# Attention by head pairs in a three-stage fp32 program: probabilities leave PSUM once, the product with V runs as plain fp32 on two column strips, and three stages share one block

## The reference, cut to what matters

```python
# q, k, v: [4 batches, 8 heads, 576, 64]
x = (log1p(|i - j|) / log1p(max(i, 1)))[..., None]
bias = maximum(x @ w1 + b1, 0) @ w2            # [576, 576, 8 heads]
scores = q @ k.T / 8 + bias
attn = exp(scores - max) / (sum(exp) + 1e-9)
x = (attn @ v) as [2304 tokens, 512]
h = x @ w_in                                    # w_in [512, 2048]
x = (maximum(h, 0) + alpha * minimum(h, 0)) @ w_out
# then a soft mixture of 8 experts with 4 slots each on x: dispatch by a softmax
# over the tokens, two layers per expert, and combine by a softmax over the slots
```

## Time and profile before

| | |
|---|---|
| median of 3 runs | 880.94 us (880.53 to 884.0) |
| the profiled execution | 884.02 us |
| its span in the profile | 882.2 us |
| PE busy | 798.5 us, 91% |
| PEld busy | 662.0 us, 75% |
| DVE busy | 557.7 us, 63% |
| ACT busy | 395.8 us, 45% |
| POOL busy | 204.6 us, 23% |
| mean granted TensorE clock | 0.964 |

### The profile page before, as it was taken

One profiled execution on the slowest core, in us unless ns is written; L12 is line 12 of the kernel. 1 busy time (PEld: TensorE's weight loads), 2 busy tenths in 40 slices (PEclk: granted clock), 3 DMA queues, 4 the chain that ended last, 5 costly groups with the idle time before them and its releaser, 6 DMA issues. The chain is left out here.

```text
span 882.2 us, 15146 instructions
## 1 busy us (share of the span) xinstructions
PE 798.5 (91%) x5068; PEld 662.0 (75%) x5068; DVE 557.7 (63%) x967; ACT 395.8 (45%) x830; POOL 204.6 (23%) x114
## 2 busy tenths in 40 slices
PE   7697889989998999689999999999999999997777
PEld 1121889989988999589899999998999999963224
DVE  6586799999999999586654354354354353354213
ACT  5586778878887888553221121121121121143212
POOL 0300845654664562300311011011011000000000
PEclk9899899999999999789999999999999999998985
DMA  9666662553642631643440040040040016750997
GB/s 358 229 178 176 239 224 91 207 184 111 227 166 107 234 122 43 147 167 131 100 97 11 1 97 10 0 93 14 0 92 15 0 50 236 275 201 1 360 350 266
DMA packets 67689, 123.72 MB, mean 140 GB/s; under 512 B 7512, under 2 KB 34024, under 8 KB 65224
## 3 DMA queue, kind: packets, MB, share of 16 engines
q1 hardware_dynamic: 60456, 113.77, 40.5%
q10 hardware_dynamic: 7200, 9.51, 3.0%
HBM read 98.42 MB, written 24.92 MB: 140 GB/s over the span
## 5 line engine op out<-in xcount | busy, mean ns | idle before, releaser
L967 ACT ACTIVATE g_hi<-g 128x384 fp32r<-128x384 f32 x96 | 50.4, 526 | 302.7 <-DVE g L922 302.7
L918 DVE TENSOR_SCALAR neg<-h,alpha 128x384 f32<-128x384 f32 x96 | 59.3, 617 | 178.1 <-PE h L882 177.5
L882 PE MATMUL h<-x_hi,w_in_hi 128*128 128x384 f32 x384 | 130.1, 339 | 6.6 <-DVE w_in_lo L935 6.6
L882 PE MATMUL h<-x_hi,w_in_lo 128*128 128x384 f32 x384 | 129.9, 338 | 0.0
L882 PE MATMUL h<-x_lo,w_in_hi 128*128 128x384 f32 x384 | 129.7, 338 | 0.0
L648 DVE CUSTOM_DVE_ANT_0 prob<-scores,bias_h 128x576 f32<-128x576 f32 x144 | 107.8, 749 | 18.6 <-PE scores L581 18.6
L695 ACT ACTIVATE prob<-prob,nmax 128x576 f32<-128x576 f32 x144 | 110.9, 770 | 7.8 <-DVE nmax L648 7.7
L896 PE MATMUL y<-w_out_hi,g_hi 128*128 128x512 f32 x288 | 112.6, 391 | 0.9 <-DVE g_lo L928 0.7
L896 PE MATMUL y<-w_out_lo,g_hi 128*128 128x512 f32 x288 | 112.7, 391 | 0.0
L896 PE MATMUL y<-w_out_hi,g_lo 128*128 128x512 f32 x288 | 112.5, 391 | 0.0
L591 PE MATMUL turned<-consts,prob 128*128 128x128 f32 x576 | 87.2, 274 | 25.1 <-DVE pt_lo L665 25.0
(11 more groups left out here) (129 smaller groups left out, 1369.6 us busy)
## 6 DMA issues: line engine op xcount, KB each, us to landing
expert_weights<-moe_w_dram SPq DMA_DIRECT2D x24, 1024.0 KB, 7.3
qk_raw<-qk_dram SPq DMA_DIRECT2D x16, 1184.0 KB, 6.2
bias_rows<-out_sb SPq DMA_DIRECT2D x40, 256.0 KB, 2.8
bias_h<-bias_rows SPq DMA_DIRECT2D x32, 288.0 KB, 3.2
x_raw<-x_parts SPq DMA_DIRECT2D x24, 384.0 KB, 5.9
expert_weights<-moe_w_dram SPq DMA_DIRECT2D x16, 512.0 KB, 8.8
v_raw<-v_dram SPq DMA_DIRECT2D x16, 320.0 KB, 5.4
x_parts<-x_out ACTq DMA_DIRECT2D x16, 288.0 KB, 2.1
```

The costliest lines, as they stand in the source:

```text
L882: last = pe.matmul(h[f % 3][:, 0:MLP_CHUNK], w[:, f, kt, :], x[:, kt, :], start=kt == 0 and x is x_hi and w is in_hi, stop=kt == d_tiles - ...
L918: dve.tensor_scalar(neg[f % 2][:], bank, 0.0, alpha[:, f:f + 1], ALU.min, ALU.mult).then_inc(neg_made, 1)
L967: act.activation(g_hi[f % 3][:], g[f % 2][:], ACT.Copy).then_inc(g_hi_made, 1)
```

## The change

Attention is done by pairs of heads for one batch, instead of one head for pairs of batches. A unit is still nine tiles (four of head a, four of head b, alternating, and one with the two rests of 64 queries), and there are still 16 units.

- The probabilities leave PSUM once, in fp32: a `take` of 128 x 512 by ScalarE for even tile numbers and by VectorE for odd ones. `pt_lo`, `low`, `low_tails` and the split of V on GpSimd are gone. The keys 512 to 575 of two neighbouring tiles (heads a and b) are turned together in one 128 x 128 transpose and leave by one VectorE copy (`take_fifth`).
- `weigh` is done five times a unit (for each pair of tiles, and the rest). Head a's product writes partitions 0 to 63, head b's 64 to 127: each matmul is plain fp32 with 64 stationary columns of V and 128 streaming queries (64 for the rest). For each of four blocks of keys there are two such matmuls, and then two with 64 rows and 64 columns for the fifth block.
- The result is x transposed, with the two heads on 128 partitions, and stays in SBUF (`xx`); `x_parts`, its loads and the addition on GpSimd are gone. The MLP's output goes back into the same tensor.
- The row sums are transposed with the tail tile and inverted as 9 x 128 on VectorE.
- All nine bias tiles of a head pair are kept; they are loaded again every fourth unit.
- The bias stage, attention and the MLP run in one block; on TensorE the first three `hidden` of the MLP stand between the last steps of attention. The first chunk of x and the first four tiles of `w_in` are split during the last three units. Loops are written out.
- The bias stage loads its table in 21 pieces, five of them at the start and then one every second step, and the other loads go between the stores.

The core of the diff:

```diff
@@ weigh, TensorE
-                    for kt in range(K_TILES):
-                        if kt == TAIL_TILE:
-                            pe.wait_ge(s_lo_tails, STEPS // 3 * m + s // 3 + 1)
-                        for pt in (pt_hi, pt_lo) if kt < TAIL_TILE else (pt_hi,):
-                            last = pe.matmul(sums[:, 0:HALF], v_st[j][:, ab * K_TILES + kt, :, :],
-                                             pt[:, kt, first:first + HALF], ...)
+            if p < PAIRS:
+                self.taken_wait(pe, n - 1)
+            self.taken_wait(pe, n)
+            pe.wait_ge(self.fifth_taken, self.groups_before(u, p) + 1)
+            for kt in range(K_TILES):
+                for x in range(2):
+                    moving = self.pt_tail[:, kt, TAIL * x:TAIL * (x + 1)] if p == PAIRS else self.pt[p % 2][:, x, kt, :]
+                    pe.matmul(self.sums[TAIL * x:TAIL * (x + 1), cols], v[:, K_TILES * x + kt, :], moving,
+                              start=kt == 0, stop=False)
+            for x in range(2):
+                own = slice(TAIL * x, TAIL * (x + 1))
+                moving = self.fifth_tail[own, own] if p == PAIRS else self.fifth[p % 2][own, :]
+                last = pe.matmul(self.sums[own, cols], v[own, 2 * K_TILES, :], moving, start=False, stop=True)
@@ out of PSUM
-                def low(m, s):
-                    dve.wait_ge(s_hi, n + 1)
-                    dve.tensor_tensor(pt_lo[...], turned[s % 2][...], pt_hi[...].bitcast(F32), ALU.subtract)
+    def take(self, eng, copy, n):
+        u, s = divmod(n, TILES)
+        eng.wait_ge(self.turned, n + 1)
+        when(eng, self.weighed, self.last_use(u, s))
+        copy(self.place_of(s), self.turn_bank[n % 2][:]).then_inc(self.taken[n % 2], 1)
@@ vector_step
+        old = n - TAKE
+            if old % 2 == 1:
+                self.take(dve, dve.tensor_copy, old)
+            if old % TILES == TAIL_TILE or old % TILES % 2 == 1:
+                take_fifth(old)
+        if n < ALL_TILES:
+            negate(n)
@@ lags
-        EXP, TURN, HI, LO, HIGH_TAILS, LOW_TAILS = 1, 3, 3, 4, 4, 4
+TURN, TAKE, WEIGH, LAST_LAG = 2, 3, 4, 5
@@ table of the bias stage
-TABLE_PIECES = (1, 2, 4, 8, 13, 13)
+TABLE_PIECES = (1, 2) + (2,) * 19
+TABLE_AHEAD = 5
@@ one block, TensorE
+                bias.tensor(pe)
+                for n in range(attention.STEPS):
+                    attention.tensor_step(pe, keep, ak, n)
+                    if n == ALL_TILES + 1:
+                        pe.wait_ge(attention.maxed, ALL_TILES)
+                    if 0 <= n - ALL_TILES - 1 < mlp.EARLY:
+                        mlp.hidden(pe, keep, weights, 0, n - ALL_TILES - 1)
+                mlp.tensor(pe, keep, weights)
@@ chunk of x for the MLP, GpSimd
-    pool.tensor_tensor(keep.x_raw[0][:], keep.x_raw[0][:], keep.x_raw[1][:], ALU.add).then_inc(keep.x_summed, 1)
-    pool.tensor_tensor(keep.x_raw[0][:], keep.x_raw[0][:], inverses, ALU.mult).then_inc(keep.x_scaled, 1)
+    pool.tensor_tensor(keep.x_raw[0][:], keep.chunk(m), keep.x_raw[1][:], ALU.mult).then_inc(keep.x_scaled, 1)
```

More of the change, by code:

```diff
@@ L219, in set_signs @@
+    for x in range(2):
+        place = ak.bias[TAIL * x:TAIL * (x + 1), TAIL_TILE].rearrange("p a b -> p (a b)")
+        sp.dma_start(place, rows[2 * hp + x, 4 * P:SEQ, :]).then_inc(ak.bias_in[t], 16)
 def set_signs(pool, keep):
@@ L1004, in experts @@
-def experts(nc, weights, w1, w2, out, mk):
-    tiles, d_tiles, f_tiles = TOKENS // P, D_MODEL // P, EXPERT_FF // P
-    chunks, in_chunk = TOKENS // MLP_CHUNK, MLP_CHUNK // P
+        self.params_in, self.prep, self.w1_ready = sem("params_in"), sem("prep"), sem("w1_ready")
+        self.x_in = [sem(f"x_in{k}") for k in range(len(TABLE_PIECES))]
+        self.hid_made = sem("hid_made")
+        self.relu_made = [sem(f"relu_made{e}") for e in range(2)]
+        self.res_made = sem("res_made")
+        self.moved = [sem(f"moved{e}") for e in range(2)]
@@ new lines, in gpsimd, with tensor, hidden, heads @@
+    def gpsimd(self, pool, ak):
+        set_signs(pool, ak)
+        split_qk(pool, ak, 0)
+    def tensor(self, pe):
+        def hidden(p):
+            s, e = p // 2, p % 2
+            if e == 0:
+                pe.wait_ge(self.x_in[self.piece_of(s)], 16)
+            if p >= 3:
+                pe.wait_ge(self.relu_made[(p - 3) % 2], (p - 3) // 2 + 1)
+            for half in range(2):
+                rows = slice(TABLE_ROWS * (2 * e + half), TABLE_ROWS * (2 * e + half + 1))
+                last = pe.matmul(self.hid[p % 3][:, half], self.w1s[rows, :], self.x_buf[rows, s, :],
+                                 start=True, stop=True)
+            last.then_inc(self.hid_made, 1)
+        def heads(s):
+            if s >= 2:
+                self.move_wait(pe, s - 2)
+            for e in range(2):
+                pe.wait_ge(self.relu_made[e], s + 1)
+            for c in range(GROUPS):
+                last = pe.matmul(self.res[s % 2][TABLE_ROWS * c:TABLE_ROWS * (c + 1), :], self.w2s,
+                                 self.hid_sb[(2 * s + c // 2) % HID_RING][:, c % 2], start=True, stop=True)
+            last.then_inc(self.res_made, 1)
+        pe.wait_ge(self.w1_ready, 1)
+        pe.wait_ge(self.params_in, 16)
+        for p in range(3):
+            hidden(p)
+        for s in range(STEPS_A):
+            for p in (2 * s + 3, 2 * s + 4):
+                if p < 2 * STEPS_A:
+                    hidden(p)
+            heads(s)
+        for s in (STEPS_A - 2, STEPS_A - 1):
+            self.move_wait(pe, s)
@@ new lines, in scalar, with relu, move @@
+    def scalar(self, act):
+        def relu(s):
+            act.wait_ge(self.hid_made, 2 * s + 1)
+            if s >= 2:
+                act.wait_ge(self.res_made, s - 1)
+            act.activation(self.hid_sb[2 * s % HID_RING][:], self.hid[2 * s % 3][:],
+                           ACT.Relu).then_inc(self.relu_made[0], 1)
+        def move(s):
+            act.wait_ge(self.res_made, s + 1)
+            if s >= OUT_RING:
+                act.wait_ge(self.stored[s % OUT_RING], 16 * (s // OUT_RING))
+            act.activation(self.out_sb[s % OUT_RING][:], self.res[s % 2][:], ACT.Copy,
+                           scale=-8.0).then_inc(self.moved[0], 1)
+        for s in range(STEPS_A + 1):
+            if s < STEPS_A:
+                relu(s)
+            if s >= 1 and not self.by_vector(s - 1):
+                move(s - 1)
@@ L1013, in experts @@
+def experts(nc, weights, d, mk):
+    tiles, d_tiles, f_tiles = TOKENS // P, D_TILES, EXPERT_FF // P
+    chunks, in_chunk = CHUNKS, MLP_CHUNK // P
+    w1, w2, out = d.w1, d.w2, d.out
     half_tiles, halves = tiles // 2, 2
@@ L1155, in second_layers @@
                                              hidden_t[half][:, P * i + SLOTS * e:P * i + SLOTS * (e + 1)],
-                                             weights[i][:, 2 + half, e, :], start=half == 0 and i == 0,
+                                             expert_tile(weights, i, 2 + half)[:, e, :], start=half == 0 and i == 0,
                                              stop=half == halves - 1 and i == 3)
@@ L1492, in routing_constants @@
                           axis=1).astype(np.float32)
+@dataclass
+class Arrays:
+    table: object
+    small: object
+    qk: object
+    v: object
+    w_in: object
+    w_out: object
+    alpha: object
+    phi: object
+    w1: object
+    w2: object
+    consts: object
+    out: object
+    bias: object
+    inverses: object
 def program(nc, table, small, qk, v, w_in, w_out, alpha, phi, w1, w2, consts, out):
     bias_rows = nc.dram_tensor("bias_rows", [HEADS, SEQ * SEQ], F32).ap()
-    x_parts = nc.dram_tensor("x_parts", [HEADS, P, TOKENS], F32).ap()
```

1355 lines of the change are left out of this document (641 added, 714 removed).

## The result

The changed kernel takes 874.5 us (median of 5 runs, 872.0 to 875.44). The kernel before, run beside it, takes 880.8 us (5 runs, 878.41 to 884.0). The ratio is 0.9923, 95% interval 0.9896 to 0.9951: it is faster by 6.3 us in the medians, where 20.8 were forecast. Between the two traces stand 12.0 us, therefore, and 5.7 of them are the scatter of these two executions (12.0 - 5.7 = 6.3, the medians' difference).

What follows compares the result with a forecast made beforehand. VectorE was taken to pace attention, TensorE close behind. Terms -2.4 - 8.2 - 5.8 - 3.5 - 2.2 + 2 = -20.1 us took 884.0 to 864; the median's distance made 861, stated as 860 us, range 830 to 882.

Steps and rivals of the forecast that it cites:

- (1): Bias stage: the wait for a store behind the loads goes, -8.2 us.
- Rival D: Bias stage: stores queue again behind `qk_raw` and the bias loads, 8.2 us not saved, 868 us; chance 0.08.
- (2): Barrier to attention: TensorE's idle 6.1 us shrink to some 0.3, -5.8 us.
- (3): Join from attention's last product to the first MLP matmul: the 6.5 us wait becomes 3, -3.5 us.
- (4): Start of the MLP: the stretch at half clock goes, -2.2 us.
- (5): Last attention units: splits of `w_in` and x moved there may delay `negate`, nothing to 6 us, taken as +2 us.
- attention, -2.4 us: Attention stage: 279 us against 281.4, with TensorE becoming the bound.
- the wait of 0.35 us a unit: Attention: TensorE waits for VectorE's copies 0.35 us, twice in every second unit.
- Changing the width: Attention's product groups: three changes of the array's width at 0.09 us each, five groups, 1.4 us a unit.
- Rival C: Attention: TensorE as the bound waits at other places, 18.2 us a unit, 875 us; chance 0.15.
- Rival B: Attention's product: the two 64-wide strips don't run abreast, 5.3 us more a unit, 945 us; chance 0.10.
- A: Attention: TensorE's unit is cheaper, middle switch free and no wait, 15.7 us a unit, 835 us; chance 0.22.

Runs made afterwards that it cites:

- e4: The kernel before with only the change's order of loads in the bias stage: 872.3 us, ratio 0.9907.
- e10: The changed kernel with the old order of loads in the bias stage: 880.31 us, ratio 1.0008 to the kernel before.
- e1: The changed kernel with V's fifth block on all 128 rows, so no change of width in the middle of a group: 861.31 us, ratio 0.9782.
- e2: The changed kernel with the fifth matmuls after the first two key tiles, four changes of width a group instead of three: 886.76 us, ratio 1.0059.
- e7: The changed kernel with the edits of e1 and e3, and the fourth pair's product directly ahead of the tail's: 851.54 us, ratio 0.969.
- e3: The changed kernel with the products one step later, every change of width kept: 869.44 us, ratio 0.9844.
- e5: The kernel before with the addition of 1e-9 to the sums of exponentials left out: 854.51 us, ratio 0.9714.
- e9: The kernel before with the new order of loads and the addition of 1e-9 moved from VectorE to ScalarE, nothing left out: 844.75 us, ratio 0.959.

## Why the prediction was off, point by point

**The bias stage, right.** The part called (1) was sized at -8.2 us. The last `res` stands at 74.19 in place of 82.51, 8.3 earlier, and no store is waited for; e4 (7.7 us less in the medians) and e10 (first score 9.1 later than in after) show that size from both sides. Rival D, stores that queue behind `qk_raw`, did not happen.

**The barrier, right.** (2) was -5.8: TensorE idles 0.75 us ahead of the first score in place of 6.12, 5.4 less. The first score was forecast near 76 and stands at 76.01.

**The join to the MLP, right in kind, taken too low.** (3) and (4) were -3.5 and -2.2, together -5.7; measured -8.1. The wait is 2.04 us where 3 were taken (6.55 - 2.04 = 4.5), the half clock is gone (2.2), and so is a wait of 0.7 in the MLP, which was no term; the rest no row names. (5), +2 for the splits, was right: one split, of x on VectorE, holds up two copies and with them TensorE, 1.7 us in one unit. The other waits of attention for VectorE's `nmax` are one, of 0.4 us. The prediction also counted two stretches of the kernel before at half clock; a third, 88.4 to 95.2 us, stands at the start of attention (granted clock 0.50), and the last one begins at 364.9, 6 us before attention ends. After has neither, and no term held what that is worth.

**The step that failed: attention, -2.4 us.** With (5) it was forecast at -0.4; it measured +10.7. The prediction wrote "TensorE's work is then 5.4 + 4.8 + 4.5 + 0.8 + 1.4 = 16.9 us a unit", and with the wait 17.25; the steady units take 18.06. The mechanism was right (TensorE is the bound, strips abreast, changes of width, waits for copies), and the wait of 0.35 us a unit was near too (0.31 measured). Mis-sized was first the term "Changing the width": 0.09 a change was read from the earlier trace rows as the gap alone, and the pass behind a change, 0.045 longer, and the first score matmul, 0.1 longer, were not read. A change costs 0.14 to 0.2, which e1, e2 and e7 confirm at 0.15, 0.15 to 0.17 and 0.34 for two. A large group was forecast at 10 x 0.112 + 0.27 = 1.39 us and took 1.83 - 0.24 = 1.59 (less the transpose and the score matmul): 0.8 us a unit on four of them. The tail's group was forecast at 1.07 in all and took that (in the timeline of after, 1.31 us from the last transpose ahead of it to the second score matmul behind it, less 0.24 for those two steps without a change), since its small passes had been taken high. Left out was second the wait for the single fifth bank, 0.15 us a unit, which e3 took away together with the other. The transposes at 0.109 in place of 0.112 give 0.13 back, the wait for the copies 0.04: 0.8 + 0.15 - 0.13 - 0.04 = 0.8, the distance from 17.25 to 18.06. Over 16 units it is 13 us. Of the 3 us that were allowed for filling the chain 1.5 were needed (292.1 less 16 x 18.06 and 1.7 for the split), and the split cost 1.7 in place of 2: 13.0 - 1.5 - 0.3 = 11.2, and attention is off by 10.7 + 0.4 = 11.1.

The Trainium skill, TensorEngine Tiling (Array Packing), Key Properties, says that changing the tiling mode drains the array while tiles of one mode work in parallel. The trace agrees with both: records 7 ns apart on two strips, and a price at each of the three changes, the one between half and quarter width too, for which no row of before had a number.

**Rival C's numbers came out, and that is luck.** It gave 18.2 us a unit and 875 us, and 18.09 and 874.5 were measured. Its reason was that TensorE waits as VectorE had. But the waits that were not forecast are 0.15 us a unit, and 0.8 are the passes and changes of width inside the groups, which e1 and e2 move by 0.15 a change. Rival B is refuted, strips of 64 are abreast; so is A, no switch is free. The turning point named for B was 1.25 us a unit above the forecast: after is 0.8 above it and still faster than before, e2 is 1.6 above it and slower.

**A rival that was missed.** The prediction read `total_eps` at 2.62 us against a least of 0.17 and booked it as one item in VectorE's relief. It asked for every term of the change what it was worth, but not what this one instruction alone was worth: 38.8 us of VectorE's time over 16 units, of which e5 turned 24.6 into shorter time before TensorE became the bound. The change removed this stall with the rest, and gave TensorE units that are 3 us longer (18.09 with waits, against 15.1). With the stall gone, the kernel before beats the changed one by 30 us (e9 against after), and both have the new order of the loads. The changed kernel can be mended too, and e7 is 23 us faster than after in the medians; it still stands at 0.969 against 0.959, with 16.47 us a unit against 15.09. By the rows the passes themselves are not the loss. The product of before is 36 matmuls of 0.133, 4.8 us a unit; the fifty passes of after are 40 of 0.109 and ten of 0.058 (64 columns), 4.9 us. What e7 still pays on top is four ways in and out of half width, 4 x 0.34 = 1.4 us, about the distance between the two periods (16.47 - 15.09 = 1.38). This sum is argued from rows; no run takes the last four away.

What the mechanism of that stall is was shown only in part. That the instruction ends with GpSimd's is in the rows, and that it costs the period is shown by e5 and e9. The addition that reads PSUM in after runs beside a GpSimd subtraction in 14 of 16 units and is not held up:

```profile
L729 DVE TENSOR_SCALAR inv_rows<-fifth_bank x16: 268/273/279, 94.4 to 365.7; 9x128 f32<-9x128 f32 x16
```

The Trainium skill, SBUF — State Buffer, Who interferes with whom, says that VectorE and GpSimd share a pair of ports as an exclusive lock, that a `tensor_scalar` is among the operations that can need the pair, and that whoever comes second is blocked for the other's whole instruction. The trace agrees: 2.33 to 2.71 us in place of 0.17 for the addition from SBUF to SBUF, ending with the other's end, against 0.27 for the one from PSUM and 0.21 for the inversion in e5. The MLP of before has a second kind: nine of its 96 `g_lo` subtractions, both inputs in SBUF, have a GpSimd operation on `x_raw` beside them, take 1.06 to 3.06 us in place of 0.55 and end 0.42 after it. That it is this lock and not another was not tried by itself.

**What stays open.** Why the first pass behind a change is 0.045 us longer, when the gap before it is already there, no run tells. A second bank for the fifth transposes, without the later lag, was not tried, nor was e7 with a shorter join to the MLP (TensorE waits 4.3 us there, and the clock is 1.2 GHz from 351.1 to 357.9). Which stages hold the 5.7 us of scatter between the two profiled executions is open too.

## What to carry to other kernels

Count for TensorE, beside the columns, each place where the shape of the array's use changes, and measure the price to the second instruction behind it: here 0.14 to 0.2 us, so that the stretch around a group of ten passes takes 1.83 us where 1.33 would do without the changes. Before a rewrite that relieves an engine, look in its tiles for an instruction whose median is far above its least, and ask what that one alone is worth: here an addition of nine columns was worth more than the rewrite. And if a change has several parts, run the cheapest one alone: the order of one queue was the whole gain.

## What the runs showed of the hardware that was not expected

- A change between full width, half width (strips of 64 columns) and quarter (64 x 64) costs TensorE about 0.14 us on the way in, 0.14 in the middle and 0.2 on the way out at full clock, part of it in the first pass behind the change (0.154 in place of 0.109).
- A VectorE addition of 128 x 9 from SBUF to SBUF took 2.33 to 2.71 us behind the start of a GpSimd operation, 15 times, and 0.17 without one; the `reciprocal` on the same columns took 0.20 to 0.21 beside the same operations (e5). A subtraction of two SBUF tiles was held up too, 3.06 us in place of 0.55 at most.
- The inversion of 9 x 128 took 0.93 us, with 128 columns, against 0.21 for 128 x 9: the columns count and not the elements.
- Twice the rows in the fifth matmuls (e1) cost nothing that shows: their four records take 0.39 us, and 0.43 on 64 rows behind a change of width.
